# Fused attention and two feed-forward layers on one core: a 192-byte SBUF tile of small values becomes 128 bytes

## The reference

```
scores = q @ k^T / sqrt(64)                  # batch 2, 8 heads, 768 positions, 64 per head
keep   = (column < 4) or (0 <= row - column < 128)
a      = softmax(where(keep, scores, -1e9))
x      = (a @ v), heads side by side         # 1536 tokens x 512
h = x @ w_in        (512 x 2048);  g = h if h >= 1, 0 if h <= -1, else (h+1)^2/4;   x = g @ w_out
h = x @ w_in2       (512 x 2048);  g = h if h > 0 else exp(h) - 1;                  out = g @ w_out2
```

## Time and profile before

| | |
|---|---|
| median of 3 runs | 648.56 us (647.56 to 648.87) |
| the profiled execution | 647.56 us |
| its span, first to last instruction | 645.9 us |
| granted TensorE clock, mean | 0.991 |
| TensorE busy | 624.1 us (97%), 4164 matmuls |
| VectorE, ScalarE, GpSimd busy | 376.0, 348.9, 74.5 us |

### The profile page before, as it was taken

One profiled execution on the slowest core, in us unless ns is written; L12 is line 12 of the kernel. 1 busy time (PEld: TensorE's weight loads), 2 busy tenths in 40 slices (PEclk: granted clock), 3 DMA queues, 4 the chain that ended last, 5 costly groups with the idle time before them and its releaser, 6 DMA issues.

```text
span 645.9 us, 12200 instructions
## 1 busy us (share of the span) xinstructions
PE 624.1 (97%) x4164; PEld 552.0 (85%) x4164; DVE 376.0 (58%) x994; ACT 348.9 (54%) x830; POOL 74.5 (12%) x147
## 2 busy tenths in 40 slices
PE   5788999999999999999999999999999999999997
PEld 3687889999999999999999988888888888888886
DVE  6799978886886788698758853222332223322221
ACT  5687756666675676666656664333443334533333
POOL 5112222320321223122000000000000000000000
PEclk8799999999999999999999999999999999999999
DMA  8664212320321232123055400000100000100001
GB/s 285 194 217 144 70 36 89 93 78 25 103 70 58 64 88 88 39 64 103 0 196 173 154 1 0 1 1 0 66 0 0 0 0 0 65 0 0 0 0 65
DMA packets 15275, 42.48 MB, mean 66 GB/s; under 512 B 2852, under 2 KB 4536, under 8 KB 15248
## 3 DMA queue, kind: packets, MB, share of 16 engines
q0 software_dynamic: 7040, 20.57, 10.6%
q1 hardware_dynamic: 8208, 21.56, 9.7%
HBM read 38.98 MB, written 3.15 MB: 65 GB/s over the span
## 4 chain that ended last, share of the span: by engine, by line
PE 86%; DVE 9%; ACT 2%; issue 1%; DMA 0%; ACTq 0%; SPq 0%; DVEq 0%
PE h_ps L507 13%; PE h_ps L508 12%; PE h_ps L509 12%; PE y_ps L522 10%; PE y_ps L524 9%; PE y_ps L523 9%; PE s_ps L524 3%; PE s_ps L523 3%; PE s_ps L522 3%; PE o_ps L490 3%; PE t_ps L470 2%; DVE wout_lo L840 1%; PE s_ps L461 1%; PE s_ps L460 1%; DVE win_lo L840 1%
## 5 line engine op out<-in xcount | busy, mean ns | idle before, releaser
L507 PE MATMUL h_ps<-x_hi,win_hi 128*128 128x256 f32 (+1 forms) x576 | 186.3, 323 | 0.8 <-DVE g_full L866 0.2
L508 PE MATMUL h_ps<-x_lo,win_hi 128*128 128x256 f32 (+1 forms) x576 | 183.2, 318 | 0.0
L509 PE MATMUL h_ps<-x_hi,win_lo 128*128 128x256 f32 (+1 forms) x576 | 183.1, 318 | 0.0
L522 PE MATMUL y_ps<-g_hi,wout_hi 128*128 128x256 f32 (+1 forms) x480 | 145.7, 304 | 2.4 <-DVE g_lo L853 2.2
L524 PE MATMUL y_ps<-g_hi,wout_lo 128*128 128x256 f32 (+1 forms) x480 | 144.8, 302 | 0.0
L523 PE MATMUL y_ps<-g_lo,wout_hi 128*128 128x256 f32 (+1 forms) x480 | 144.7, 301 | 0.0
L870 DVE SCALAR_TENSOR_TENSOR g_full<-g_full,h_ps 128x512 f32<-128x512 f32 x48 | 33.0, 688 | 156.5 <-ACT g_full L675 156.5
L507 PEld LDWEIGHTS h_ps<-x_hi,win_hi 128*128 128x128 f32 x576 | 109.0, 189 | 11.1 <-DVE g_full L866 1.2
L509 PEld LDWEIGHTS h_ps<-x_hi,win_lo 128*128 128x128 f32 x576 | 108.8, 189 | 8.7
L508 PEld LDWEIGHTS h_ps<-x_lo,win_hi 128*128 128x128 f32 x576 | 108.9, 189 | 8.7
L662 ACT CAST g_hi<-g_full 128x256 fp32r<-128x256 f32 (+1 forms) x144 | 68.5, 476 | 71.9 <-DVE g_full L866 37.4
(11 more groups left out here) (109 smaller groups left out, 818.4 us busy)
## 6 DMA issues: line engine op xcount, KB each, us to landing
ks<-in_k POOLq DMA_DIRECT2D x40, 260.0 KB, 2.9
raw<-in_w_in SPq DMA_DIRECT2D x11, 512.0 KB, 4.2
raw<-in_w_out SPq DMA_DIRECT2D x11, 512.0 KB, 3.5
qs<-in_q POOLq DMA_DIRECT2D x40, 128.0 KB, 2.7
vals<-in_v POOLq DMA_DIRECT2D x20, 192.0 KB, 3.0
out_y<-xy SPq DMA_DIRECT2D x12, 256.0 KB, 2.1
xy<-in_w_in SPq DMA_DIRECT2D x5, 512.0 KB, 4.6
xy<-in_w_out SPq DMA_DIRECT2D x5, 512.0 KB, 3.7
```

Of the source, the lines that this page charges most:

```text
L507: pe.matmul(o, win_hi[:, k, f], x_hi[:, k, :], start=(k == 0), stop=False)
L508: pe.matmul(o, win_hi[:, k, f], x_lo[:, k, :], start=False, stop=False)
L509: last = pe.matmul(o, win_lo[:, k, f], x_hi[:, k, :], start=False, stop=(k == KT - 1))
L522: pe.matmul(o, wout_hi[:, t, cols], g_hi[:, t % GR, :], start=begin, stop=False, skip_group_check=True)
```

## The change

The tile `small` is asked for with 32 columns instead of 48. The views into it stay where they were, `half` in column 16 among them, so what is left out is 16 of the columns that nothing names.

```diff
-        small = sb("small", [P, 3 * IN_FLIGHT * 4 * QB])
+        small = sb("small", [P, 2 * IN_FLIGHT * 4 * QB])
```

## The result

| | before | after |
|---|---|---|
| median of 9 runs | 647.56 us (645.57 to 648.87) | 652.0 us (650.91 to 654.3) |
| ratio to before | 1 | 1.0077 (95% interval: 1.0057 to 1.0096) |
| span of the profiled execution | 645.9 us | 649.1 us |

The kernel became slower by 0.8%, beyond the range's upper end of 651.0. Before and after ran the same instructions in the same order.

The account below looks back on a forecast made before the run. The prediction took the time as the number of matmuls times their pace on a full TensorE, plus a start. Terms of 0 left 647.56 us; the shown runs' median, 1.0 us above, gave 648.5 us, range 646.0 to 651.0.

Parts of the forecast that it names:

- What bounds the kernel: Whole kernel: TensorE busy 624.1 of 645.9 us; other engines set the end of anything only up to 110 us.
- What the change takes away and moves: Whole kernel: no instruction or wait goes, 0 us; every tile behind small begins 64 bytes earlier.
- The term of the matmuls: 3,456 matmuls of both layers with shifted moving tiles: 0 us, outer bound 5.2 us either way, smallest step 1.4 us.
- Rival A: Both layers: weights and moving operand reads hinder each other, a tick lost per matmul, 1.4 us, 650.0 us; chance 0.07.
- Rival B: Second layer's 512-column matmuls pay for their place and would gain 5.6 us, 642.9 us; chance 0.03, mild form 0.04.
- VectorE and ScalarE: Their reads and writes of shifted tiles: 0 us, bounds 2.1 us and 0.8 us either way.
- The sign that I had named for L572: ScalarE's L572 into probs and xy: medians still 27 ns apart would show that this was never a matter of place.
- DMAs: First transfer, of qs and ks, the only landing waited for: 0 us, bounds 0.2 us either way.
- The range: Whole kernel: 646.0 to 651.0 us, from the runs' spread plus 1.4 us to either side, the outer bounds left outside.

Follow-up runs that it names:

- only_moving_back: Changed kernel with only the first layer's x_hi, x_lo, g_hi and g_lo padded back 64 bytes to their bytes of before; 1.0012 of before.
- distance_192: Changed kernel with small at 80 columns, so the tiles behind it lie 192 bytes further; 0.9983 of before.
- distance_0: Changed kernel with small at 64 columns, so the tiles behind it lie 128 bytes further; 0.9992 of before.
- second_layer_at_128: Kernel before with 64 bytes of padding ahead of the second layer's tiles alone; 640.37 us, 0.9911 of before.
- all_but_moving_back: Changed kernel with ramp, g_full, attention tiles and masks back at their bytes of before, the first layer's moving tiles not; 1.0124 of before.

## Why the prediction failed

| kernel | shift, first layer | ns, 256 columns | first layer, us | shift, second | ns, 512 columns | second layer, us | ratio |
|---|---|---|---|---|---|---|---|
| before | 64 | 115.2 | 348.6 | 64 | 233.3 | 268.6 | 1 |
| after | 0 | 118.8 | 354.4 | 0 | 232.4 | 267.5 | 1.0077 |
| only_moving_back | 64 | 115.3 | 348.1 | 0 | 233.3 | 268.6 | 1.0012 |
| distance_192 | 192 | 117.8 | 352.5 | 192 | 228.9 | 263.5 | 0.9983 |
| distance_0 | 128 | 119.6 | 355.6 | 128 | 226.7 | 260.9 | 0.9992 |
| second_layer_at_128 | 64 | 115.2 | 348.6 | 128 | 226.7 | 260.9 | 0.9911 |

(Paces and layers from the starts of the matmuls' rows: the first layer from its first feed-forward matmul to the first of 512 columns, the second from there to the last. The first layers of before and second_layer_at_128 contain about 1.0 us at the lower clock, the others none.)

**What bounds the kernel** was right, and it is why 4 ns count: TensorE is full from 110 us on, in both kernels.

**What the change takes away and moves** was right: nothing runs differently, and the 64 bytes are all.

**The term of the matmuls** is the step that failed. I took 0, with 5.2 us as the outer bound and 1.4 as the smallest step. Measured are 5.8 us in the first layer, some 6.8 at an equal clock by the estimate above (8.0 of pace, less about 1.1 of shorter waits) and 6.3 against only_moving_back, which ran at one, and -1.1 in the second. The outer bound was 1.5 ns for a matmul; the first layer's lost 3.6. Two errors are in it. First, I took the rows of the scores for a test of place. They test the place of the moving operand on a 64-byte grid, and what counts is the distance to the weights by 256 bytes. A shift of 64 leaves the grid alone and changes that distance by a quarter of its period. Second, I read the pace off twelve matmuls at 302 us, and took it for the pace. 50 us further on the same rows show 117.5 ns. Two paces for one kind of matmul, at one clock and with no waits inside the stretches, were a sign in the trace of before that something else than the columns sets it, and I didn't ask what.

**Rival A** named what the runs point to: weights and moving operand read at the same time, their distance going from 64 to 128 within 256. That the distance counts is shown, how the two reads meet is not. Its price was a tick, 0.42 ns; it is 3.6 ns in 2,304 matmuls and about -0.9 in 1,152. I had given it 0.07. **Rival B** was right in that the 512-column matmuls pay for their place, and wrong in where the good place is: at shift 128 they give back 7.3 us, which is more than the 5.6 forecast, and at the change's shift 0 only 1.1.

**VectorE and ScalarE**: the term of 0 holds. L809 and L603 after:

```profile
L603 ACT ACTIVATE probs<-s_ps,small x80: 458/469/482, 32.5 to 319.4; 128x260 f32<-128x260 f32 x80
...
L809 DVE TENSOR_SCALAR probs<-probs,small x80: 346/354/361, 35.0 to 320.7; 128x260 f32<-128x260 f32 x80
```

as in the earlier trace rows, and all_but_moving_back shows no loss from their tiles' places. The sign that I had named for L572 tells nothing: its two medians, 27 ns apart before, are 420 and 462 ns after, but its rows lie in the first 30 us, where the clocks of the two executions differ. **DMAs**: the first transfer took 2.05 us in the chain after, against 2.37. These are two single executions, so whether the place has a part in the 0.3 us can't be told, and the kernel became slower all the same. **The range** was built by keeping the outer bound of the matmuls outside, on the word of one row. With it the range would have held.

## What to carry to other kernels

Where TensorE is full and each matmul loads its own weights, the place of tiles in SBUF is a parameter like any other: by padding alone the pace went from 113.3 to 120.0 ns at 256 columns and from 226.7 to 234.6 at 512 with TensorE alone, and from 115.2 to 119.6 and from 226.7 to 233.3 in the whole kernel. So when a tile's size changes, look at what it pushes along, and compare the starts of matmuls, not their durations, in several stretches of the trace. A price for place is read only from rows that differ in the distance between the two operands, and a pad is worth trying for each width by itself; a kernel with TensorE alone and many places gives a whole table in one run.

## What the runs showed of the hardware

- The pace of matmuls of fp32r data (the type of the split float32 operands) depends on the distance between moving operand and weights in SBUF, with a period of 256 bytes: sixteen places and the same sixteen 256 bytes on agree within 0.02 us of 17. The Trainium skill (TensorE: Matmul & The Clock Gate, Step-by-step: what each phase is for) says that loading the next tile's weights doesn't steal read bandwidth from the running matmul. These runs show that the place of the next weights does change the pace: with TensorE alone, 256-column matmuls take 116.7, 117.8 or 120.0 ns as the next weights lie at distances 192 and 64 in turn, at 64, or at 0, each at two different sets of distances to their own weights. Whether that is read bandwidth, and how the two reads meet inside, is not shown.
- At one distance (64) and 256 columns there are two steady paces, 113.3 and 117.8 ns, each of which can last for 96 matmuls and more. With TensorE alone, scores left the slow one and transposes and `values` the fast one, twice each. In the kernel before, 26 of 40 stretches behind scores ran at the fast one, and at 330 us a gap of 0.49 us between two starts, with no other matmul between, was followed by 39 us at the slow one.
- At 512 columns distance 0 to both the own and the next weights gives 226.7 ns, the fastest measured; with only one of the two at 0 it was 231.7. At 256 columns that distance is the slowest, 120.0.
- A slower TensorE waits less, but here not by much: between only_moving_back and the changed kernel, both at a clock of 1.00 in the first layer, 3.5 ns in each of 2,175 intervals are 7.6 us of lost pace, and about 1.1 came back in shorter intervals around waits (59 of them, 17.0 and 15.9 us).
